# Hash-masked attention with two expert stages: row sums in another layout, the bias in another form, and the preparation of q and k moved within a step

## What is computed

```python
q_bits = (np.einsum('bhsd,dk->bhsk', q, proj) > 0)     # 6 bits a row; the same for k
mask = q_bucket[:, :, :, None] == k_bucket[:, :, None, :]
scores = np.where(mask, scale * np.matmul(q, k.transpose(0, 1, 3, 2)), -1e9)
scores = scores - np.max(scores, axis=-1, keepdims=True)
attn = np.exp(scores)
attn = attn / (np.sum(attn, axis=-1, keepdims=True) + 1e-09)
return np.matmul(attn, v)
```

## Time and profile before

| | |
|---|---|
| median of 3 runs | 1020.56 us (1018.45 to 1023.21) |
| the profiled execution | 1019.28 us, its span 1017.7 us |
| PE busy | 916.4 us, 90% of the span |
| DVE busy | 603.0 us, 59% |
| ACT busy | 500.0 us, 49% |
| POOL busy | 471.8 us, 46% |

### The profile page before, as it was taken

How to read it: one execution, slowest core, us unless ns; L and a number is a source line. 1 busy time by engine, 2 the same in 40 slices (tenths; PEclk the granted TensorE clock), 3 DMA queues, 4 the chain that set the end, 5 groups by cost and what they waited for, 6 DMA issues and landing times.

```text
span 1017.7 us, 17832 instructions
## 1 busy us (share of the span) xinstructions
PE 916.4 (90%) x5505; PEld 787.9 (77%) x5506; DVE 603.0 (59%) x1229; ACT 500.0 (49%) x886; POOL 471.8 (46%) x373
## 2 busy tenths in 40 slices
PE   5598888888896499999999999998489999999998
PEld 4477777777785388888888888887379999999997
DVE  6498898888977332222232222231289878878776
ACT  3466766767764122222222222221167777777775
POOL 4543443444444454563655536430467655453221
PEclk9799999999998699999999999999699999999999
DMA  9745424433233666887786767933522020100000
GB/s 202 223 145 139 102 77 123 104 97 100 73 143 123 223 226 214 283 256 217 251 285 210 243 208 232 312 126 114 163 96 63 25 70 21 52 22 19 32 1 31
DMA packets 88149, 143.63 MB, mean 141 GB/s; under 512 B 15522, under 2 KB 47778, under 8 KB 87586
## 3 DMA queue, kind: packets, MB, share of 16 engines
q1 hardware_dynamic: 46450, 72.19, 23.8%
q0 software_dynamic: 19328, 54.53, 16.7%
q10 hardware_dynamic: 22320, 16.26, 5.4%
HBM read 123.30 MB, written 19.66 MB: 140 GB/s over the span
## 4 chain that ended last, share of the span: by engine, by line
PE 69%; DVE 10%; issue 8%; POOL 6%; ACT 2%; DMA 2%; SPq 2%; ACTq 0%; DVEq 0%; POOLq 0%
PE ps_s L1105 17%; PE ps_o L1130 17%; PE ps_s L1173 13%; PE ps_t L1159 6%; DVE mx L1262 3%; PE ps_m L1159 3%; PE ps_s L1159 3%; PE ps_s L1116 3%; PE ps_t L987 2%; PE ps_o L1000 2%; POOL qs L595 2%; DVE den L1274 2%; POOL tile_t L592 1%; PE ps_s L978 1%; DVE km L1254 1%
## 5 line engine op out<-in xcount | busy, mean ns | idle before, releaser
L552 POOL TENSOR_TENSOR w_r<-raw,w_r 128x1024 f32 (+1 forms) x72 | 171.7, 2401 | 103.9 <-DMA raw<-in_moe_w 45.8
L1105 PE MATMUL ps_s<-w_r,xT 128*128 x744 | 179.6, 398 | 17.0 <-DVE xT L1476 17.0
L1130 PE MATMUL ps_o<-w_r,hT 128*128 x744 | 175.6, 393 | 2.6 <-DVE hT L1480 2.6
L1105 PEld LDWEIGHTS ps_s<-w_r,xT 128*128 128x128 f32 x744 | 139.4, 191 | 45.0 <-issue 17.2
L1130 PEld LDWEIGHTS ps_o<-w_r,hT 128*128 128x128 f32 x744 | 140.8, 189 | 32.1 <-issue 2.8
L1173 PE MATMUL ps_s<-w_r,g_r 128*128 128x512 f32 x576 | 145.4, 398 | 4.4 <-DVE g_r L1562 4.4
L1486 DVE COPY y_sb<-ps_o 128x512 f32<-128x512 f32 x31 | 21.4, 692 | 211.5 <-PE ps_o L1130 211.5
L1173 PEld LDWEIGHTS ps_s<-w_r,g_r 128*128 128x128 f32 x576 | 107.7, 190 | 24.8 <-issue 4.1
L691 POOL TENSOR_TENSOR m<-q,g_r 128x384 f32<-128x384 f32 x64 | 66.0, 1031 | 114.4 <-DVE g_r L1550 114.1
L835 ACT ACTIVATE hT<-ps_s 128x1024 fp32r<-128x1024 f32 x31 | 31.8, 1026 | 160.2 <-DVE y_sb L1486 116.4
L750 ACT ACTIVATE prob<-ps_s,nb,sc 128x768 f32<-128x768 f32 x96 | 95.1, 991 | 28.4 <-DVE nb L1267 27.4
(11 more groups left out here) (245 smaller groups left out, 1525.7 us busy)
## 6 DMA issues: line engine op xcount, KB each, us to landing
w_r<-in_moe_w POOLq DMA_DIRECT2D x32, 1024.0 KB, 8.0
raw<-in_moe_w SPq DMA_DIRECT2D x56, 512.0 KB, 3.9
q_in<-in_q SPq DMA_DIRECT2D x56, 176.0 KB, 3.5
k_in<-in_k SPq DMA_DIRECT2D x56, 176.0 KB, 4.3
xg<-x_slots ACTq DMA_DIRECT2D x124, 64.0 KB, 3.1
y_slots<-y_sb ACTq DMA_DIRECT2D x31, 256.0 KB, 4.2
raw<-in_moe_w SPq DMA_DIRECT2D x16, 256.0 KB, 2.9
raw<-in_moe_w_in SPq DMA_DIRECT2D x8, 512.0 KB, 5.0
```

What stands on the lines that cost most here:

```text
L552: pool.tensor_tensor(of_chunk(buf, 1, n), raw[:, par, :], of_chunk(buf, 0, n).bitcast(F), ALU.subtract).then_inc(split_done, 1)
L1105: mm = pe.matmul(ps_s[0][:, o * 512:o * 512 + 512], xT[:, par, part, c * P:c * P + P], w_r[:, buf, wpart, col:col + 512], start=(c == 0 an ...
L1130: mm = pe.matmul(ps_o[:, :], hT[:, part, c * P:c * P + P], w_r[:, buf, wpart, col:col + DM], start=(c == 0 and part == 0 and wpart == 0), ...
```

## The change

1. `rs` and `den` go from the shape [P, T, 2] to [P, 2, T]. The two row sums of a step, which lay side by side, now lie six numbers apart, in what `den` reads and writes and in what `rinv` reads. The number of elements is the same.
2. `nb` is the product of `mx`, `sc` and -1 as before. It was a tensor_scalar with `mx` as its tensor and `sc` as a scalar per partition; it is a scalar_tensor_tensor with both as tensors and -1 as the scalar.
3. The tables: the tiles are turned on DVE at point 2 of steps 0, 1, 2 and 3 (behind both row maxima; before at points (0,0), (1,1), (2,2), (4,0)), rounded on ACT at point 0 of steps 1, 2, 3 and 4. The hash products of tile r stand on PE at points 0 and 2 of step 2+r, their bits on DVE at points 1 and 2 of the same step. At point 2, DVE does the bits ahead of the turning.

```diff
-    rs = small("rs", [P, T, 2], F)
-    den = small("den", [P, T, 2], F)
+    rs = small("rs", [P, 2, T], F)
+    den = small("den", [P, 2, T], F)
...
-    TURN_AT = {(0, 0): 0, (1, 1): 1, (2, 2): 2, (4, 0): 3}
-    ROUND_AT = {(0, 1): 0, (1, 2): 1, (3, 0): 2, (4, 1): 3}
-    BITS_AT = {(1, 0): 0, (1, 1): 1, (2, 1): 2, (2, 2): 3, (3, 2): 4, (4, 0): 5, (5, 0): 6, (5, 1): 7}
+    TURN_AT = {(0, 2): 0, (1, 2): 1, (2, 2): 2, (3, 2): 3}
+    ROUND_AT = {(1, 0): 0, (2, 0): 1, (3, 0): 2, (4, 0): 3}
+    PE_BITS_AT = {(2 + r, 2 * half): 2 * r + half for r in range(4) for half in range(2)}
+    DVE_BITS_AT = {(2 + r, 1 + half): 2 * r + half for r in range(4) for half in range(2)}
...
-                               scale=sc[:, i:i + 1], accum_out=rs[:, t, hh:hh + 1]).then_inc(exp_done[hh], 1)
+                               scale=sc[:, i:i + 1], accum_out=rs[:, hh, t:t + 1]).then_inc(exp_done[hh], 1)
...
-                if (t, pt) in BITS_AT:
-                    bits(n + 1, 1 - par, BITS_AT[t, pt])
+                if (t, pt) in PE_BITS_AT:
+                    bits(n + 1, 1 - par, PE_BITS_AT[t, pt])
...
-                dve.tensor_scalar(nb[:, i:i + 1], mx[:, i:i + 1], sc[:, i:i + 1], -1.0, ALU.mult,
-                                  ALU.mult).then_inc(soft_ready[hh], 1)
+                dve.scalar_tensor_tensor(out=nb[:, i:i + 1], in0=mx[:, i:i + 1], scalar=-1.0, in1=sc[:, i:i + 1],
+                                         op0=ALU.mult, op1=ALU.mult).then_inc(soft_ready[hh], 1)
...
-                dve.tensor_scalar(den[:, t, :], rs[:, t, :], 1e-9, None, ALU.add).then_inc(den_done, 1)
+                dve.tensor_scalar(den[:, :, t], rs[:, :, t], 1e-9, None, ALU.add).then_inc(den_done, 1)
                 dve.wait_ge(den_done, e)
-                dve.reciprocal(rinv[:, t, :], den[:, t, :]).then_inc(rinv_done, 1)
+                dve.reciprocal(rinv[:, t, :], den[:, :, t]).then_inc(rinv_done, 1)
...
+                if (t, pt) in DVE_BITS_AT:
+                    bits(n + 1, 1 - par, DVE_BITS_AT[t, pt])
                 if (t, pt) in TURN_AT:
                     turn_tile(n, TURN_AT[t, pt])
-                if (t, pt) in BITS_AT:
-                    bits(n + 1, 1 - par, BITS_AT[t, pt])
```

## The result

The changed kernel takes **1007.5 us** (median of 4 runs, 1006.98 to 1007.81) where the kernel before takes 1020.83 (median of 4, 1018.45 to 1023.21): ratio 0.9869, with a 95% interval of 0.9845 to 0.9892, 1.3% faster. The profiled execution has a span of 1006.0 us against 1017.7.

The account below looks back on a forecast made before the run. It took PE and DVE to be both nearly full in the attention; its terms summed to -0.4 us a pair, -2.8 in seven, plus 0.5 in the last pair, from 1020.6 to 1018, rounded down to 1017; range 994 to 1031.

Parts of the forecast that it names:

- hash products later: PE's wait for POOL's low part of q goes, and DVE's idle time behind it: -1.8 us a pair.
- `den` moved: `den`, now behind bits and turning at a step's end, mostly escapes POOL's holds: -3.4 us a pair.
- `nb` by itself: The two-tensor form of `nb` is 0.06 us shorter, twelve times a pair: -0.7 us.
- `nb` held, turning waits: POOL's operations hold the two-tensor `nb`, and the k tile's turning waits for `tile_split`: +4.6 us a pair.
- uneven load: DVE is overfull in steps 2 and 3, and PE can't use the light steps 0 and 1: +0.9 us a pair.
- What holds DVE soon holds PE: In the attention pairs, both engines nearly full: a head's scores wait for the exponential before; no separate size.
- The floor of 30.7 us a pair: PE's steps without preparation, 27.9 us, plus sixteen hash products at about 0.18 each: some 30.7 us a pair.
- The walk: Timing of a q tile from its scores of A: POOL's start and `nb` both at S + 2.2; holds 2.6 to 6.4.
- the slow rival: POOL starts on a q tile just ahead of `nb`: holds 6.4, +1.4 us a pair, 1031 us; chance 0.17.
- `nb` not held: POOL does not hold the new `nb`, only the turning waits: -3.2 us a pair, 997 us; chance 0.14.
- The layout that frees `den`: The strided `den` is no longer held by POOL: 0.5 us a pair less than forecast, 1014 us; chance 0.19.
- POOL winning the ties: POOL's first operation on a q tile precedes the `nb` of A: +1.4 us a pair, 1031 us; chance 0.17.

Follow-up runs that it names:

- e5: The kernel before with only the change's new places for hash products and their bits: 1005.77 us, ratio 0.988.
- e9: e1 with the reciprocal read straight from the row sums, leaving out the adding of 1e-9 that makes `den`: 983.76 us, ratio 0.9637.
- e11: e1 with the edits of both e9 and e10: 980.64 us, ratio 0.9605.
- e1: The changed kernel with `nb` as a tensor_scalar again, layout and tables as changed: 994.27 us, ratio 0.9735.
- e4: The kernel before with the two-tensor `nb` alone: 1043.28 us, ratio 1.0218.
- e2: The changed kernel with `rs` and `den` as [P, T, 2] again: 1007.61 us, ratio 0.9861.
- e3: The kernel before with `rs` and `den` as [P, 2, T] alone: 1020.3 us, ratio 0.9991.
- e8: e1 with the two scalars of the tensor_scalar for `nb` swapped: 989.13 us, ratio 0.9718.
- e7: e1 with the first tile turned and rounded in step 0, as in the kernel before: 989.36 us, ratio 0.9716.
- e10: e1 with the first tile turned and rounded in step 0, only in the pairs after the first: 990.85 us, ratio 0.9705.

## Why the prediction was right, and where it was not

The range of 994 to 1031 us holds the result, and "faster" was the likeliest of the three outcomes; the forecast of 1017 is 9.5 us too high, and by its own bound of 0.5% it would have been called no change. Step by step, a pair:

| term | predicted | measured |
|---|---|---|
| hash products later | -1.8 | -1.94 (e5, alone: -1.82) |
| `den` moved | -3.4 | -3.52 |
| `nb` by itself | -0.7 | -0.65 |
| `nb` held, turning waits | +4.6 | +4.03 + 0.44 = +4.5 |
| uneven load | +0.9 | about 0, at most 0.34 |
| sum | -0.4 | -1.64 (by the landmark -1.65) |

**The step that failed is the uneven load.** It stood in the ledger at its upper bound, 0.9 of "0 to 0.9", with the reason that PE can't use what DVE leaves in the light steps. What the trace shows is that DVE leaves next to nothing: all its waits for PE in the five pairs come to 1.1 + 0.4 + 0.2 = 1.7 us, 0.34 a pair. That is the most that the term can be, against 0.9. DVE's work is 30.3 us a pair by the prediction's count; with 2.1 of idle time and 3.9 of `den` the kernel before comes to 36.3, 0.7 short of its 36.97. The changed pair is 30.3 - 0.65, with 4.03 + 0.44 of `nb` and turning, 0.12 of idle time ahead of q's bits and 0.34 of `den` (6 x 57 ns over the 158 of rows 9): 34.6, short of 35.32 by the same 0.7. That balance leaves no room for a new loss of 0.9 either. The reason is argued and not tried by itself: an engine that is late all the time evens out its own load, since the scores for its light step lie ready when it gets there. The term is worth 6.3 us in the forecast's seven pairs; the four others erred by 0.14, 0.12, 0.13 and, for `nb` by itself, 0.05 the other way, some 2 us together. The lower bound is given as -1.6 a pair, but its terms (-1.8 - 3.4 - 0.7 + 4.4) make -1.5.

**Seven times the loop's pair** is the second step that failed, and luck hid it. The forecast took pairs 0 and 6 to gain what the others do and added 0.5 for the last. Pair 0 gained 7.87 us and not 1.64, most of it because its first low part of q comes late, which the steady pairs don't show; pair 6 lost 2.85; the last pair lost 2.7, with only one `nb` above 0.21 us, at 0.22, so not by the holds for which the 0.5 stood. With the 0.94 ahead of pair 0 these come to within 0.2 us of what two more pairs like the steady ones would have given. Otherwise a forecast with every term of the pair right would have been off by several us.

**What holds DVE soon holds PE**, the prediction said, through the exponentials, and one of its signs of being right was that PE's waits move there. They did not: the wait for the exponentials fell from 9.5 to 0.2 us and that for bits rose from 3.8 to 12.7. DVE's lateness reaches PE through the hash products. The floor of 30.7 us a pair (its own figures, 27.9 + 16 x 0.18, make 30.8) was too low as well: e9 and e11 stop at 31.93 and 31.78, with PE busy 31.7 of the 31.93 in e9.

**The holds of `nb`**, read from one operation of 48 elements, are shown twice: 1.63 us a pair in e1, 21 us of the whole in e4. The walk put POOL's first operation and the `nb` of A at the same point, and there they fall: in three pairs running POOL started 0.02 to 0.03 us ahead (98.16 and 98.19 above; 133.95 and 133.97; 169.25 and 169.27). So POOL did win those ties, the condition of the slow rival, and the price of 6.4 was still wrong. The second q tile, for which up to 1.8 had been allowed, held one `nb` of each pair, for 0.26 to 0.82 us.

**The wait for `tile_split`** was put at 1.8 alone and at nothing where `nb` is held as long. Both are shown: 8.7 us in five waits in e1, and in the changed kernel a single wait, of 2.0 us. It comes in the one pair in which POOL began 1.2 us ahead of the `nb` of A, so that `nb` was hardly held:

```profile
204.77 1.47 POOL L593 TENSOR_TENSOR tile_t<-tile_t,qscale 64x768 f32<-64x768 f32 x1 [12.49 <-ACT qs L784]
205.97 0.28 DVE L1268 SCALAR_TENSOR_TENSOR nb<-mx,sc 128x1 f32<-128x1 f32 x1
208.25 0.98 DVE L1241 STREAM_TRANSPOSE tile_t<-k_in 128x768 f32<-128x768 f32 x1 [2.00 <-POOL qs L596]
```

**The rivals.** `nb` not held (997) fell: mean 496 ns. e1 is the kernel in which it is not, and checks the arithmetic: 997, with 7 x 0.65 for the dearer form and without 7 x 0.9 for the uneven load, is 995, and e1 took 994.27. (From 1020.6 - 7 x 3.2 the rival's own figure would be 998, one more than it says, and the sum goes over seven equal pairs here too.) The layout that frees `den` (1014) fell in e2 and e3. POOL winning the ties (1031) was right in its condition and wrong in its price. By the rule of the Trainium skill (VectorE: DVE Perf Modes, section "Mode 2×_2P"), which asks that the outermost dimension be even, or odd and equal in source and destination, and says nothing of the step, the new `den` should take both ports like the old, and so be held like it; the traces agree, 215 ns against 214 in e2 and 797 against 801 in e3. The forecast was said to fall as a whole if a pair took under 35 us with `nb` held; it took 35.32.

On the hold itself the Trainium skill (SBUF — State Buffer, section "SBUF: two separate sides") says that a VectorE operation with two SBUF inputs and a GpSimd operation that reads SBUF exclude each other for the whole instruction: whichever starts first goes ahead. The trace agrees down to one element a partition, where POOL is first: `nb` at 98.19 ends 0.02 us after the POOL operation at 98.16. The other order no row here shows.

## What to carry to other kernels

Before replacing a one-tensor form on VectorE by a two-tensor form that reads 54 ns faster, look at what GpSimd does at that time: here twelve tiny operations a pair were held 4 us for a gain of 0.65, and going back to the old form made the pair 1.63 us shorter. Where one engine is busy throughout, make the ledger on that engine alone and enter an uneven load at zero, unless its idle time shows in the light steps. Read the first and the last turns of a loop by themselves: here pair 0 gained nearly as much as the five after it together. Move a producer and its consumer together, and test each move on both orders: the turnings' new places brought 1.5 us a pair behind the new products, and cost some 33 us of the whole with the old ones.

## What the runs showed of the hardware that was not expected

- A tensor_scalar on two elements that lie six apart is held by GpSimd just like one on two neighbours (797 and 801 ns in the mean, single ones up to 2265).
- A scalar_tensor_tensor on a single element a partition is held too, up to 1918 ns where it takes 160 alone; a tensor_scalar on the same element, with the second number as a scalar from memory, never is (96 of 96 between 212 and 216 ns in the kernel before, in e1 and in e8), whichever of its two scalars that is.
- q's loads held the turnings where the pair had become shorter and the first tile was still turned at point 0 of step 0: 4.8 us in e5 (pairs of 35.15 us), 4.3 in e7 and 2.8 in e10, and none in the kernel before with the same place and pairs of 36.97. With the tile at point 2 there is none either, not even in e9 with pairs of 31.93. What holds the loads back there is not shown.
